# First pair of an attention and expert kernel: parts split ahead of the transposes, loads on one queue, two expert weights loaded later

## The reference, cut to what matters

```python
def _attn_ref(q, k, v):                       # (4, 8, 1152, 64) each, float32
    q_pool = q.reshape(B, H, S // 2, 2, D).mean(axis=3)
    scores = (1.0 / np.sqrt(D)) * np.matmul(q_pool, k.transpose(0, 1, 3, 2))
    scores = scores - np.max(scores, axis=-1, keepdims=True)
    attn = np.exp(scores)
    attn = attn / (np.sum(attn, axis=-1, keepdims=True) + 1e-09)
    return np.matmul(attn, v)
```

## Time and profile before

| what | value |
|---|---|
| median of 3 runs | 830.46 us (829.24 to 831.13) |
| the profiled execution | 830.63 us |
| its span, first to last instruction | 828.6 us |
| TensorE busy | 796.7 us |
| DVE busy | 502.6 us |
| ACT busy | 466.8 us |
| GpSimd busy | 174.6 us |
| mean granted TensorE clock | 0.988 of full speed |

### The profile page before, as it was taken

One profiled execution on the slowest core, in us unless ns is written; L12 is line 12 of the kernel. 1 busy time (PEld: TensorE's weight loads), 2 busy tenths in 40 slices (PEclk: granted clock), 3 DMA queues, 4 the chain that ended last, 5 costly groups with the idle time before them and its releaser, 6 DMA issues. The chain is left out here.

```text
span 828.6 us, 17284 instructions
## 1 busy us (share of the span) xinstructions
PE 796.7 (96%) x5747; PEld 603.5 (73%) x5747; DVE 502.6 (61%) x966; ACT 466.8 (56%) x896; POOL 174.6 (21%) x233
## 2 busy tenths in 40 slices
PE   4999999999999999999999999998999999999997
PEld 3777777777777777777777777763334788888875
DVE  6657666666566566665765766745124566666664
ACT  4766666766666667666676676642014453334342
POOL 3431422413314224133141340000000330000000
PEclk9999999999999999999999999999999799999999
DMA  7937365383473652834636518546999001010011
GB/s 247 269 88 181 74 150 118 90 192 85 114 171 73 155 114 85 199 83 117 156 81 162 113 30 226 223 152 266 380 393 384 5 1 51 0 52 14 39 51 26
DMA packets 83000, 112.03 MB, mean 135 GB/s; under 512 B 45328, under 2 KB 47376, under 8 KB 82448
## 3 DMA queue, kind: packets, MB, share of 16 engines
q1 hardware_dynamic: 82544, 110.91, 47.3%
q10 hardware_dynamic: 416, 0.59, 0.2%
HBM read 71.37 MB, written 4.72 MB: 92 GB/s over the span
## 5 line engine op out<-in xcount | busy, mean ns | idle before, releaser
L534 PE MATMUL scores<-k_stack,q_stack 128*128 128x384 f32 x960 | 274.5, 376 | 0.6 <-ACT probs L674 0.6
L479 PE MATMUL tbank<-ident,probs 128*128 128x128 f32 x1296 | 220.3, 279 | 4.3 <-DVE pt L816 2.5
L702 ACT COPY pt<-tbank 128x384 f32<-128x384 f32 x256 | 122.9, 480 | 144.1 <-PE tbank L479 142.9
L479 PEld LDWEIGHTS tbank<-ident,probs 128*128 128x128 f32 x1296 | 156.7, 140 | 61.1 <-issue 40.4
L674 ACT ACTIVATE probs<-scores,neg_max 128x1152 f32<-128x1152 f32 x144 | 176.0, 1222 | 8.1 <-PE tbank L479 2.1
L761 DVE TENSOR_REDUCE row_max<-scores 128x1 f32<-128x384 f32 x144 | 80.1, 556 | 129.3 <-PE scores L534 127.4
L569 PE MATMUL obank<-pt,v_in 128*64 128x256 f32 x1152 | 148.8, 389 | 0.0
L534 PEld LDWEIGHTS scores<-k_stack,q_stack 128*128 128x128 f32 x960 | 147.7, 191 | 1.2 <-ACT probs L674 1.0
L754 DVE TENSOR_REDUCE row_max<-scores 128x1 f32<-128x768 f32 x144 | 136.7, 949 | 4.0 <-PE scores L534 1.3
L569 PEld LDWEIGHTS obank<-pt,v_in 128*64 128x64 f32 x1152 | 72.8, 136 | 49.3 <-issue 23.5
L332 POOL TENSOR_TENSOR k_hi<-k_lo,one 128x512 fp32r<-128x512 f32 (+1 forms) x45 | 37.2, 826 | 297.9 <-ACT k_lo L619 277.0
(11 more groups left out here) (202 smaller groups left out, 768.3 us busy)
## 6 DMA issues: line engine op xcount, KB each, us to landing
weights<-in_moe_w SPq DMA_DIRECT2D x7, 2048.0 KB, 12.4
v_in<-in_v SPq DMA_DIRECT2D x16, 576.0 KB, 4.1
k_in<-in_k SPq DMA_DIRECT2D x30, 288.0 KB, 4.9
k_stack<-k_hi SPq DMA_DIRECT2D x30, 288.0 KB, 3.6
k_stack<-k_lo SPq DMA_DIRECT2D x30, 288.0 KB, 3.5
q_in<-in_q SPq DMA_DIRECT2D x15, 512.0 KB, 4.8
q_stack<-q_hi SPq DMA_DIRECT2D x30, 144.0 KB, 3.3
q_stack<-q_lo SPq DMA_DIRECT2D x30, 144.0 KB, 3.9
```

The costliest lines, as they stand in the source:

```text
L479: last = nc.tensor.transpose(tbank[:, bank, cols], src, ident[0:rows, 0:rows])
L534: last = nc.tensor.matmul(scores[:, bank, 0:CH], q_stack[at.par][:, h, order, cols], k_stack[at.par][:, h, keys], start=(x == 0), stop=(x ...
L702: nc.scalar.copy(pt_out(at, e), tbank[:, bank_of(at, e), 0:3 * P].rearrange("p (r q) -> p r q", r=3)).then_inc(out_by_act, 1)
```

## The change

The first pair is made in another way.

- **Loads.** All of pair 0's loads stand on SP's queue, one DMA for each head: keys of head 0, queries of head 0, keys of head 1, queries of head 1, both tails; then pair 1's keys. ACT issues none.
- **Parts.** High and low are made ahead of the transposes, in `k_parts` and `q_parts`. Keys: ACT rounds, DVE subtracts (`first_keys_high`, `first_keys_low`). Queries (`first_queries`): four operations for each group, the full sum, the rounded sum twice and the difference. DVE makes the first tile of both heads; GpSimd starts only when DVE has finished those, and makes tile 1 of both heads, the tails, then tiles 2 and 3.
- **Transposes.** What is copied out of PSUM is then the finished stack, one copy each. There are 38 transposes instead of 28, since queries are transposed in both orders. Head 0's keys and first query tile come first; head 1's follow behind tile 0's scores, and tiles 1, 2, 3 and the tails at four places in periods 1 to 3 (`FIRST_AT`). Five matmuls of the identity with itself are added ahead.
- **SP's wait** for loading pair 1's queries to `q_in` is now for GpSimd's last query part.
- **Early weights.** The two 2 MB loads move from SP's start to its body of the second pair, behind that pair's stack copies and values load.

```diff
@@ SP @@
         for h in range(2):
             sp.dma_start(k_stage[:, h]..., k_v[:, h]...).then_inc(k_staged[h], 16)
+            sp.dma_start(q_in[:, h, 0:NF, :]..., q_full[:, h, :]).then_inc(q_loaded[0] if h else q_first_in, 16)
+        sp.dma_start(q_in[0:TAIL, :, NF, :], q_tail[:, 0:2, :]).then_inc(q_loaded[0], 16)
+        for h in range(2):
+            sp.dma_start(k_in[:, 1, :, h, :], k_v[:, 2 + h]).then_inc(k_loaded[1], 16)
         load_keys(At(0), 1)
         load_values(At(0), 0)
         load_values(At(0), 1)
-        for n in range(EARLY):
-            mem.load_weight(sp, n)
...
             if at.pair + ahead == 1:
-                sp.wait_ge(q_twice_v, 2)
-                sp.wait_ge(q_twice_p, 2)
+                sp.wait_ge(q_parts_v, 2)
+                sp.wait_ge(q_parts_p, 3)
...
+            if at.step is None and at.pair == 1:
+                for n in range(EARLY):
+                    mem.load_weight(sp, n)
@@ queries @@
+    def first_queries(engine, ops, tiles, heads, rows, step, summed, done):
+        halves = [q_in[0:rows, heads, tiles, a:a + D] for a in (0, D)]
+        total = q_total[0:rows, heads, tiles, :]
+        ops.tensor_tensor(total, *halves, ALU.add).then_inc(summed, 1)
+        ops.tensor_tensor(q_parts[0:rows, heads, tiles, 0, :], *halves, ALU.add).then_inc(summed, 1)
+        ops.tensor_tensor(q_parts[0:rows, heads, tiles, 2, :], *halves, ALU.add).then_inc(summed, 1)
+        engine.wait_ge(summed, 3 * step)
+        ops.tensor_tensor(q_parts[0:rows, heads, tiles, 1, :].bitcast(FP32), total,
+                          q_parts[0:rows, heads, tiles, 0, :].bitcast(FP32), ALU.subtract).then_inc(done, 1)
@@ GpSimd @@
-        pool.wait_ge(k_staged[1], 16)
-        double_keys(nc.gpsimd, 1, slice(0, NK)).then_inc(k_twice_p, 1)
-        double_queries(pool, nc.gpsimd, 1, q_twice_p)
+        pool.wait_ge(q_parts_v, 2)
+        first_queries(pool, nc.gpsimd, 1, slice(0, 2), P, 1, q_hi_p, q_parts_p)
+        first_queries(pool, nc.gpsimd, NF, slice(0, 2), TAIL, 2, q_hi_p, q_parts_p)
+        first_queries(pool, nc.gpsimd, slice(2, NF), slice(0, 2), P, 3, q_hi_p, q_parts_p)
@@ TensorE @@
+        FIRST_AT = {(0, 2): ("A1", "q1", "B1", "E1"), (1, 0): ("tile1",), (1, 2): ("tile2",),
+                    (2, 2): ("tile3",), (3, 2): ("tail",)}
+        def first_transposes(name):
+            if name in ("A0", "B0"):
+                pe.wait_ge(k_lo_first, 1 + (name == "B0"))
+            elif name == "A1":
+                pe.wait_ge(k_lo_first, 3)
+            elif name in ("q0", "q1"):
+                pe.wait_ge(q_parts_v, 1 + int(name[1]))
+            elif name == "tile1":
+                pe.wait_ge(q_parts_p, 1)
+                pe.wait_ge(first_by_dve, 2)
+            elif name == "tile2":
+                pe.wait_ge(q_parts_p, 3)
+                pe.wait_ge(first_by_dve, 4)
...
+        for n in range(5):
+            nc.tensor.matmul(obank[:, 0:P], ident[:], ident[:], start=True, stop=True)
+        for name in ("A0", "B0", "q0", "E0"):
+            first_transposes(name)
@@ ACT @@
+        first_keys_high(0, slice(0, 4))
+        first_keys_high(0, slice(4, NK))
+        first_keys_out(act, nc.scalar.copy, "A0", first_by_act)
+        first_keys_high(1, slice(0, NK))
+        for name in ("B0", "E0", "A1"):
+            first_keys_out(act, nc.scalar.copy, name, first_by_act)
@@ DVE @@
+        first_keys_low(1, 0, slice(0, 4))
+        first_keys_low(2, 0, slice(4, NK))
+        dve.wait_ge(q_first_in, 16)
+        first_queries(dve, nc.vector, 0, 0, P, 1, q_hi_v, q_parts_v)
+        dve.wait_ge(q_loaded[0], 32)
+        first_queries(dve, nc.vector, 0, 1, P, 2, q_hi_v, q_parts_v)
+        first_query_out(0)
+        first_keys_low(3, 1, slice(0, NK))
...
                 if at.pair == 0 and t == 0:
-                    first_low(6)
+                    first_query_out(1)
+                    for name in ("B1", "E1"):
+                        first_keys_out(dve, nc.vector.tensor_copy, name, first_by_dve)
+                if at.pair == 0 and t in (1, 2):
+                    first_tile_out(dve, nc.vector.tensor_copy, f"tile{t + 1}", first_by_dve)
+                if at.pair == 0 and t == 3:
+                    first_tail_out()
```

More of the change, by code:

```diff
@@ L339, in split @@
         last.then_inc(lo_ready, 1)
[L341 to L354, removed]
@@ new lines, in first_keys_out, with first_tile_out @@
+    def first_keys_out(engine, copy, name, done):
+        a, b = KEYS[name[0]]
+        engine.wait_ge(first_ready, first_done(name))
+        copy(k_stack[0][:, int(name[1]), P * a:P * b], FIRST_BANK[name][:, 0:P * (b - a)]).then_inc(done, 1)
+    def first_tile_out(engine, copy, name, done):
+        i = int(name[4])
+        engine.wait_ge(first_ready, first_done(name))
+        copy(q_stack[0][:, :, :, P * i:P * i + P],
+             FIRST_BANK[name].rearrange("p (h o c) -> p h o c", h=2, o=2)).then_inc(done, 1)
@@ L579, in pair @@
                         score_chunk(at, t, j)
+                    if at.pair == 0:
+                        for name in FIRST_AT.get((t, j), ()):
+                            first_transposes(name)
                     if (t, j) in EXTRA:
@@ L588, in _ @@
         pe.wait_ge(zeros_ready, 2)
[L589 to L602, removed]
-                    rows = min(P, width - m)
-                    tile = NF if rows == TAIL else (cols.start + m) // P
-                    src = (k_twice if what == "k" else q_twice)[0:rows, h, tile].rearrange("p a d -> p (a d)")
-                    last = nc.tensor.transpose(bank[:, at + m:at + m + rows], src, ident[0:rows, 0:rows])
-            last.then_inc(first_ready, 1)
+        for n in range(5):
+            nc.tensor.matmul(obank[:, 0:P], ident[:], ident[:], start=True, stop=True)
+        for name in ("A0", "B0", "q0", "E0"):
+            first_transposes(name)
         each_pair(pe, pair, ends=(NPAIR,))
@@ L706, in pair @@
                         softmax_exp(at, *((0, t - 1) if t else (1, NTILE - 1)))
+                        if at.pair == 0 and t == 1:
+                            first_tile_out(act, nc.scalar.copy, "tile1", first_by_act)
                     if (t, j) in EXTRA and EXTRA[t, j] in PREP_BY_ACT:
@@ L721, in _ @@
             nc.vector.memset(q_stack[par][:, 1, :, NF * P:SQ].bitcast(FP32), 0.0).then_inc(zeros_ready, 1)
-        def first_low(n):
-            h, part = FIRST[n]
-            bank = FIRST_BANKS[n]
-            dve.wait_ge(first_hi, n + 1)
-            for what, cols, at in first_pieces(h, part):
-                width = cols.stop - cols.start
-                if what == "k":
-                    low = [(slice(D, 2 * D), k_stack[0][D:2 * D, h, cols])]
-                else:
-                    low = [(slice(D, 2 * D), q_stack[0][D:2 * D, h, 0, cols]),
-                           (slice(0, D), q_stack[0][0:D, h, 1, cols])]
-                for rows, half in low:
-                    last = nc.vector.tensor_tensor(half, bank[rows, at:at + width], half.bitcast(FP32), ALU.subtract)
-            if part in "EC":
-                last.then_inc(first_stack, 1)
@@ L828, in pair @@
                         maxima(at, t)
-                        if at.pair == 0 and t == 1:
-                            first_low(7)
                 if at.pair < NPAIR:
```

121 lines of the change are left out of this document (75 added, 46 removed).

## The result

The changed kernel takes 822.94 us (median of 20 runs, 820.70 to 827.73). Twenty runs of the kernel before have a median of 827.35 (824.61 to 831.76), not the 830.46 of the first three. The ratio is 0.9943, 95% interval 0.9925 to 0.9962: 4.7 us gained by the ratio (the two medians differ by 4.4), with 3.1 to 6.2 inside the interval. The forecast was 4.0 us, 826.5 us, with a range from 823.8.

A forecast was written before the change was run, and what follows sets the result against it. TensorE, busy 96%, was taken as the bound, with a chain from GpSimd's query parts to pair 1's stack copies setting the gain: 830.63 less 4.0 = 826.6, or 826.5 against the median of 830.46; range 823.8 to 829.9.

The forecast's parts named there:

- The base: Start of the sum: 830.63 us of the profiled execution (828.6 span and 2.03 around it), beside the median of 830.46.
- The mark's place: First score matmul of pair 1's second tile, taken at 47.24, 1.26 us after its last stack copy lands.
- T: Time at which GpSimd has finished its query parts of pair 0: 14.0 us, bounds 12.4 and 23.
- T to the mark: From GpSimd's last query part through pair 1's query load, sums, splits and stack copies to its second tile: 29.25 us.
- TensorE ahead of the mark: TensorE arrives at pair 1's second tile before the stack copies: a new wait of 0.5 to 1.7 us.
- Q0: TensorE's step ahead of pair 1's second tile, needing GpSimd's sums: about 20.5 to 21.3 against 26.27.
- The weights: Moving two early weight loads behind pair 1's stack copies and values: zero, at most 11.47 us without that cover.
- The first: Chain to pair 1's second tile faster than priced, TensorE sets its start: gain 6.2, 824.3 us; chance 0.20.
- The second: Wait at pair 1's second tile lowers the clock again, 1.4 us each fall: gain 2 to 2.6, 828.2; chance 0.15.
- The third: GpSimd's query parts become the bound through interfaces shared with DVE: 5 us late, 835.5; chance 0.08.
- The fourth: One queue delivers no earlier than two, query operations cost more: gain 1.3, 829.2, no difference seen; chance 0.14.

The follow-up runs named there:

- e1: The kernel before, unchanged, run once more: 827.09 us, ratio 1.0000.
- e7: The changed kernel without the five matmuls on the identity: 823.20 us, ratio 0.9944.
- e3: The kernel before with only the two early weight loads moved: 829.49 us, ratio 1.0008.
- e2: The changed kernel with the two early weight loads back at SP's start: 829.60 us, ratio 1.0016.
- e4: The changed kernel, but DVE's parts of head 1's first tile don't wait for the tails' load, only GpSimd does: 822.53 us, ratio 0.9934.
- e11: The kernel before with unused identity matmuls in three places behind attention where TensorE waits: 827.55 us, ratio 0.9981.
- e12: The changed kernel with unused identity matmuls in three places behind attention where TensorE waits: 822.31 us, ratio 0.9924.

## Why the prediction was right and wrong

**The base: the step that failed.** "Sum: 830.63 of the profiled execution [...] less 4.0 = 826.6; against the median of 830.46, 826.5." The subtraction was sound and the minuend wasn't. The profiled execution had the lower clock, 830.63 us at 0.988; the three runs known then have no clock on record, but their 829.24 to 831.13 lie about where e1's three runs at 0.988 lie (829.8 to 831.3). Twenty runs give 827.35. Taken from that, the same 4.0 us give 823.4, within 0.5 us of what was measured. The base was off by 3.1 us, the gain by some 0.7 (4.7 against 4.0). And the range was made of rivals about the first 50 us alone, with no term for what one kernel's executions differ by, although the trace showed it: the windows of 0.58 and 0.90 at 640 to 660 stood in it, the one 7 in the page's row of the clock, and the mean clock of 0.988. I looked at the granted clock only around the change. What the runs show in its place is the time from the end of attention to the end of the span: 274.9 and 274.8 us in the two traces with the fall at 640 to 650 (the first of before, e7), 269.1 to 271.4 in the twelve others. It is one fall in one place: the stretch that holds it took 12.09 and 11.98 us with it, and 7.74 to 7.77 in the eight traces that have this place without the fall or the added matmuls, so that it cost some 4.3. Behind it all fourteen traces take 176.6 to 176.8. The rest of the differences, 2.0 us, lies between the end of attention and that place, and what makes it stays open: the other falls of these traces, to 0.79 to 0.87 in windows between 570 and 590, don't show in it, six of the twelve have them. Why a fall comes in some executions and not in others no run here tells either; TensorE waited 1.2 us ahead of the place in those with the fall and in those without.

**The mark's place.** The row at 47.24 in the earlier trace rows is still the third chunk of pair 1's first tile; the second tile's first is the 47.92 shown above. I had given TensorE 1.26 us of slack against the chain, where it had 1.94, and counted from 0.68 too early.

**T.** Forecast 14.0, measured 15.26. The start of GpSimd was 8.29, not 6.9: the tail landed at 7.4 and not at 5.7, the middle that I took between 4.8 and 6.52. Both bounds were too early; five issues on one queue end later than on two. The twelve operations took 6.97 (7.1 with the 0.2 for contention); the one that ran beside DVE's 576 columns took 0.97 in place of 0.45, so that the price was 0.5 and not 0.2.

**T to the mark.** Forecast 29.25, measured 44.42 - 15.26 = 29.16. That the sum held to 0.1 us is partly luck: T to the first stack copy took 14.61 and not 15.1, since GpSimd's splits ran with hardly a gap, the first to the last issue 42.56 - 29.87 = 12.69 and not 11.85, since one issue in between took 1.80, and the last issue to the mark 1.86 and not 2.3. So the gain at the mark is 4.0 + 0.68 - 1.26 + 0.09 = 3.5: the errors in the mark's place and in T partly cancelled.

**TensorE ahead of the mark.** A new wait of 0.5 to 1.7 us for the stack was forecast, 0.83 came. Q0 was forecast at 20.5 to 21.3, it came at 21.51, after a wait of 1.02 for the sums that the text had as a condition. The matmuls on the identity took 2.47 us, more than the 1.1 to 2.1 forecast, and still ended ahead of the first transpose at 4.53; they cost and gave nothing, as forecast (e7).

**The weights.** Moved, they cost nothing, as said. "Its going gives nothing" was wrong: it is true of the kernel before (e3) and false behind the faster front, where their old place costs 7.5 us (e2). I priced each part against the schedule of before, and not against the one that the other parts make.

**The rivals.** The first (TensorE sets the mark) is refuted by the bracket at 44.42 and by e4, where a shorter chain moved the mark at once. The second (a fall of the clock behind the new waits) didn't happen; the window of after that answers to the earlier trace rows reads

```profile
21.00:22.00 1.00, 0.49 (x5) 1.00 0.85 272
```

and the granted clock was 1.00 from 20 to 25 and in the windows of 10 us up to 60, so also behind the wait at the mark. The third (GpSimd the bound) had the right row and the wrong reach: one operation of twelve was hindered. The fourth was right that one queue delivers no earlier than two, and wrong that this eats the gain.

**What stays open.** Traces put the change at 3.4 to 3.5 us at the end of attention (4.4 against e1's execution) and 3.8 over the span with falls gone; timed runs put it at 4.7, 3.1 to 6.2. The interval takes in both. The medians of e11 and e12 hint at 1 us or more in the expert stage; the traces don't show it (see e1). Among runs at a clock of 0.994 or more, the medians of before and of e7 on its chip differ by 3.3 us, those of before and of e12 on its chip by 4.6. So what makes the timed gain larger than the traced one isn't shown. Nor does a run take back the splitting ahead of the transposes or the one queue alone; the experiments show what limits their gain.

## What to carry to other kernels

Before a sum is subtracted from a profiled execution, look at the granted clock over its whole span: a stretch below 1.00 far from the change may belong to that execution alone, and the forecast starts from the time without it or holds both in its range. Find the chain outside the busy engine that arrives last at the place where the gain must be taken over, price it link by link with durations of the kernel before, and check which tile the mark's row belongs to by counting its neighbours. Price the parts of a change together: a part that is worth nothing alone can be what keeps another's gain.

## What the runs showed of the hardware

- The first transposes ran at half their later rate while the granted clock printed 1.00. At 4.53 eight took 1.97 us and one 0.42, a step of (1.97 - 0.42) / 7 = 0.22 us; at 13.10 four took 0.60 and one 0.27, a step of 0.11. By these rows the column doesn't show the lower level at the start of the program; the matmuls' own step does.
- A second queue saves issue time, and that can be seen. The tail's answers among the DMA issues of the first 12 us (work, queue, count, KB, us from issue to landing), before and after:

```profile
q_in<-in_q ACTq DMA_DIRECT2D x1, 64.0 KB, 5.2
```
```profile
q_in<-in_q SPq DMA_DIRECT2D x1, 64.0 KB, 4.8
```

  Issued at 1.25 by ACT it landed at 6.45, issued fifth by SP at 2.59 it landed at 7.39: 1.34 later on its way, 0.94 later there. The Trainium skill, DMA: Bandwidth & Descriptors, Issuing engines are not separate DMA queues, says that issuing from several engines saves only the issuing time and that this is usually small beside the transfer. The rows agree with the first half; here the tail's landing, behind four other loads, set GpSimd's start (e4). No run changed the number of queues alone.
- Behind two weight loads of 2 MB each, SP's next two issues of keys took 8.88 us in after, 13.29 in before (11.47 of it the second) and 14.78 in e2; two such issues with no weights ahead of them took 2.49 in after, at 17.59. The edit of e3 takes nothing but the weights away from this place of the kernel before: the same two issues took 2.29.
